# Twelve inverse sets of one pair of chunks each, all split over partitions, in place of two split sets and five whole ones

## What is computed

```python
for t in range(S):
    y[:, :, t] = np.einsum('bhd,bhde->bhe', rt, state)
    Sa = np.einsum('bhde,bhe->bhd', state, at)
    state_decay = state * wt[:, :, None, :] - np.einsum('bhd,bhe->bhde', Sa, bt)
    state = state_decay + np.einsum('bhd,bhe->bhde', vt, kt)
```

## Time and profile before

| what | value |
|---|---|
| median of 3 runs | 884.25 us (879.71 to 886.81) |
| profiled execution | 889.22 us, its span 887.5 us |
| busy share | PE 90%, DVE 57%, ACT 44%, POOL 33% |
| POOL in the chain that ended last | 10% of the span, all ahead of 144 us |
| attention ends, gated layers start | about 450 us |

### The profile page before, as it was taken

The page is one execution under the profiler, slowest core; times in us unless marked ns, Lnnn a source line. Parts: engine busy times, 40 slices in busy tenths (PEclk is TensorE's granted clock), DMA queues, the critical chain, the costliest instruction groups (busy, mean ns, idle before and its releaser), DMA issues.

```text
span 887.5 us, 29938 instructions
## 1 busy us (share of the span) xinstructions
PE 794.7 (90%) x13477; PEld 733.7 (83%) x13477; DVE 508.2 (57%) x706; ACT 386.3 (44%) x521; POOL 291.1 (33%) x476
## 2 busy tenths in 40 slices
PE   4776887998998989788789999999999999999997
PEld 4775876887887878677678999899988999899997
DVE  5794664675665753323238658644686347853475
ACT  1223333334334334434448256731767217671374
POOL 4088894780971961840003020122002120030200
PEclk9798998899899978969999999999999999999999
DMA  9996983875795444362333000100101001010001
GB/s 114 142 137 117 115 113 84 109 105 121 95 134 88 77 115 92 86 156 41 79 87 106 1 36 1 63 1 1 37 19 45 1 0 37 19 45 1 1 1 44
DMA packets 238203, 59.10 MB, mean 67 GB/s; under 512 B 228448, under 2 KB 233468, under 8 KB 238076
## 3 DMA queue, kind: packets, MB, share of 16 engines
q1 hardware_dynamic: 160092, 43.75, 25.8%
q10 hardware_dynamic: 77984, 13.45, 11.2%
HBM read 43.01 MB, written 14.16 MB: 64 GB/s over the span
## 4 chain that ended last, share of the span: by engine, by line
PE 69%; POOL 10%; issue 6%; DVE 6%; ACT 4%; DMA 3%; ACTq 1%; SPq 1%; DVEq 0%; POOLq 0%
PE p L1045 37%; PE p L690 12%; PE p L848 3%; PE p L788 3%; POOL prod L439 3%; POOL y_t L442 3%; PE p L1137 3%; PE p L798 2%; POOL prod L456 2%; POOL t_pair L459 2%; PE p L814 2%; PE p L833 2%; PE p L711 2%; DVE stage L1340 2%; PE p L755 2%
## 5 line engine op out<-in xcount | busy, mean ns | idle before, releaser
L456 POOL TENSOR_TENSOR prod<-t_pair 128x30 f32<-128x30 f32 (+9 forms) x150 | 91.8, 612 | 92.9 <-DMA t_pair<-m_scratch 81.3
L1354 POOL TENSOR_TENSOR big<-stage,big 128x1024 fp32r<-128x1024 f32 x12 | 28.8, 2398 | 276.8 <-DVE stage L1294 276.8
L1045 PE MATMUL p<-xs,w 128*128 128x384 f32 x560 | 110.2, 335 | 0.0
L1045 PE MATMUL p<-wsg_hi,big 128*128 128x384 f32 x384 | 98.6, 335 | 2.2 <-ACT stage L1199 1.9
L1045 PEld LDWEIGHTS p<-xs,w 128*128 128x128 f32 x560 | 98.5, 188 | 0.6 <-ACT stage L1191 0.2
L1045 PE MATMUL p<-wo,big 128*128 128x320 f32 x576 | 91.4, 312 | 7.0 <-DVE big L1258 7.0
L1045 PEld LDWEIGHTS p<-wo,big 128*128 128x128 f32 x576 | 85.3, 188 | 12.3 <-DVE big L1258 11.1
L459 POOL TENSOR_TENSOR t_pair<-t_pair,prod 128x30 f32<-128x30 f32 (+9 forms) x150 | 90.2, 601 | 11.8
L1045 PEld LDWEIGHTS p<-wsg_hi,big 128*128 128x128 f32 x384 | 69.6, 188 | 3.2 <-ACT stage L1199 2.6
L616 DVE TENSOR_TENSOR ar_sb<-p,mask 128x512 f32<-128x512 f32 x24 | 16.6, 692 | 69.3 <-PE p L788 69.3
L1340 DVE SCALAR_TENSOR_TENSOR stage<-tmp,cols,stage 128x768 f32<-128x768 f32 x48 | 48.7, 1015 | 12.9 <-ACT stage L1232 12.0
(11 more groups left out here) (154 smaller groups left out, 1696.9 us busy)
## 6 DMA issues: line engine op xcount, KB each, us to landing
raw_r<-in_r_dram SPq DMA_DIRECT2D x48, 80.0 KB, 3.7
vp<-in_v_dram ACTq DMA_DIRECT2D x96, 40.0 KB, 2.6
x_scratch<-y_t ACTq DMA_DIRECT2D x48, 80.0 KB
out_dram<-stage SPq DMA_DIRECT2D x11, 320.0 KB, 2.3
m_scratch<-n_t SPq DMA_DIRECT2D x48, 64.0 KB
t_pair<-m_scratch SPq DMA_DIRECT2D x5, 512.0 KB, 4.8
t_scratch<-t_pair SPq DMA_DIRECT2D x5, 512.0 KB, 3.9
t_sb<-t_scratch SPq DMA_DIRECT2D x20, 128.0 KB, 2.7
```

Of the source, the lines that this page charges most:

```text
L456: pool.tensor_tensor(p_v, tp[:, 0:s, s:s + 1].to_broadcast([PAIRS, s, n]), tp[:, s:s + 1, s + 1:C].to_broadcast([PAIRS, s, n]), ALU.mult). ...
L1045: last = pe.matmul(out_of(p, half), l, r, start=step == 0 and first, stop=step == steps - 1 and not part)
L1354: pool.tensor_tensor(dst, src, hi.bitcast(F32), ALU.subtract).then_inc(sem_, 1)
```

## The change

Every set is now a split one with one pair of chunks: `SETS` is 12, `set_of(u)` is (u // 2, u % 2), and set g belongs to chunks 2g and 2g+1. Sets take turns in two buffers of `t_pair`, of a new `t_half` (the rows that a partition updates), of `t_sb`, and in two halves of each DRAM scratch. SP no longer loads the halved rows from DRAM; POOL copies them out of `t_pair` with two copies of 64 partitions x 512 elements at the head of each set. The two whole-matrix loads of sets 0 and 1 stay as they are; from set 2 on, a set g+2 is loaded right behind the way of set g into `t_sb`, in step 2g+7. In the steps up to 6, SP loads w (ahead of b), and the first such load of a comes behind the load of set 0. The wait of DVE ahead of the first write of `y_t` is gone.

```diff
-        SPLIT = 2
-        SETS = NU // 4 + 1
+        SETS = NU // 2
+        ELIM = [(2 * (C - 2) + 4) * g for g in range(SETS + 1)]
...
-            def next_pair(u):
+            def next_wkb(u):
                 if u % 2 == 1 and u // 2 + 2 < NU // 2:
+                    if u < R_LAG:
+                        sp.wait_ge(w_full, u + 1)
+                        load(w, "w", u // 2 + 2, w_in)
...
+            def load_set(g):
+                sp.wait_ge(m_out, 64 * (g + 1))
+                for half in range(2):
+                    sp.dma_start(t_pair[half * HP:(half + 1) * HP, g % 2], in_scratch(m_pairs, g)).then_inc(m_in, 16)
+
+            def next_a(u):
+                if u % 2 == 1 and u // 2 + 2 < NU // 2:
                     sp.wait_ge(a_full, u + 1)
                     load(a, "a", u // 2 + 2, a_in)
...
-                    if g and at == 0:
-                        sp.wait_ge(m_in, M_IN[g])
+                    if g >= 2 and at == 0:
+                        sp.wait_ge(m_in, M_IN[g - 1])
...
+                    if at == 1 and g < 2:
+                        load_set(g)
+                    if u == 1:
+                        next_a(u)
...
                     sp.wait_ge(elim, ELIM[g + 1])
-                    if g:
-                        sp.wait_ge(t_in, g * 64)
+                    if g >= 2:
+                        sp.wait_ge(t_in, T_IN[g - 1])
+                    for half in range(2):
+                        sp.dma_start(in_scratch(t_pairs, g).rearrange("n (i x) t -> x n i t", x=2)[half],
+                                     t_half[half * HP:(half + 1) * HP, g % 2]).then_inc(t_out, 16)
...
+                    if g + 2 < SETS:
+                        load_set(g + 2)
...
-            for g in range(SPLIT):
+            for g in range(SETS):
+                mine, pivot = t_half[:, g % 2], t_pair[:, g % 2]
+                done = ELIM[g]
                 pool.wait_ge(m_in, M_IN[g + 1])
+                if g >= 2:
+                    pool.wait_ge(t_out, T_OUT[g - 1])
+                for half in range(2):
+                    rows = slice(half * HP, (half + 1) * HP)
+                    if done:
+                        pool.wait_ge(elim, done)
+                    pool.tensor_copy(mine[rows], pivot[rows, half:C:2, :]).then_inc(elim, 1)
+                    done += 1
...
-            for g in range(SPLIT, SETS):
...
-                if un is not None and un % 2 == 1 and un // 2 + 2 < NU // 2:
-                    load_side(w, "w", un // 2 + 2, w_in)
+                uw = un if c is not None else u if u == R_LAG else None
+                if uw is not None and uw % 2 == 1 and uw // 2 + 2 < NU // 2:
+                    load_side(w, "w", uw // 2 + 2, w_in)
...
-                    if cy == 0:
-                        dve.wait_ge(t_out, T_OUT[SPLIT])
-                    elif cy % 2 == 0:
+                    if cy and cy % 2 == 0:
                         dve.wait_ge(y_out, 16 * 4 * (cy // 2))
```

More of the change, by code:

```diff
@@ L45, in attention_memory @@
         t.r_t = sb("r_t", [P, RR, 2, 4, 2, 2, 2, C])
-        t.t_sb = sb("t_sb", [P, 2, 4, 2, 4, C])
+        t.t_sb = sb("t_sb", [P, 2, 2, 2, 4, C])
+        t.t_half = sb("t_half", [P, 2, C // 2, C])
         t.vp = sb("vp", [P, RV, 2, H, HP])
@@ L151, in attention_part @@
     e_inv, e_end, e_t, a_t, kb_t, kb_n, n_t, r_t = mem.e_inv, mem.e_end, mem.e_t, mem.a_t, mem.kb_t, mem.kb_n, mem.n_t, mem.r_t
-    t_pair, prod, t_sb, vp, x_sb, z, s_sb, vp_t = mem.t_pair, mem.prod, mem.t_sb, mem.vp, mem.x_sb, mem.z, mem.s_sb, mem.vp_t
+    t_pair, t_half, prod, t_sb = mem.t_pair, mem.t_half, mem.prod, mem.t_sb
+    vp, x_sb, z, s_sb, vp_t = mem.vp, mem.x_sb, mem.z, mem.s_sb, mem.vp_t
     ar_sb, y_t, ident, mask = mem.ar_sb, mem.y_t, mem.ident, mem.mask
@@ L203, in attention_part @@
         y_out = sem("y_out")
-        SPLIT = 2
-        SETS = NU // 4 + 1
[L206 to L210, removed]
+        SETS = NU // 2
+        ELIM = [(2 * (C - 2) + 4) * g for g in range(SETS + 1)]
+        T_OUT = [32 * g for g in range(SETS + 1)]
+        M_IN = [32 * g for g in range(SETS + 1)]
+        T_IN = [64 * g for g in range(SETS + 1)]
         m_pairs = m_dram.rearrange("n c s t -> (n c) s t")
@@ L228, in set_of, with in_scratch @@
         def set_of(u):
[L230 to L236, removed]
+            return u // 2, u % 2
         def first_chunk(g):
-            return 2 * g if g < SPLIT else 4 * (g - SPLIT) + 4
-        def half_rows(g, rows=slice(0, P)):
-            return free(y_t[rows], g * (C // 2) * C, [[C, C // 2], [1, C]])
+            return 2 * g
+        def in_scratch(scratch, g):
+            return scratch[g % 2 * HP:g % 2 * HP + HP]
         def last_use(u):
@@ L436, in _ @@
                     p_v = prod[:, 0:m * n].rearrange("p (j t) -> p j t", t=n)
-                    if done:
-                        pool.wait_ge(elim, done)
-                    pool.tensor_tensor(p_v, t_half[:, 0:m, s:s + 1].to_broadcast([P, m, n]),
-                                       t_pair[:, g % 2, s:s + 1, s + 1:C].to_broadcast([P, m, n]), ALU.mult).then_inc(elim, 1)
+                    pool.wait_ge(elim, done)
+                    pool.tensor_tensor(p_v, mine[:, 0:m, s:s + 1].to_broadcast([P, m, n]),
+                                       pivot[:, s:s + 1, s + 1:C].to_broadcast([P, m, n]), ALU.mult).then_inc(elim, 1)
                     pool.wait_ge(elim, done + 1)
-                    pool.tensor_tensor(t_half[:, 0:m, s + 1:C], t_half[:, 0:m, s + 1:C], p_v, ALU.add).then_inc(elim, 1)
+                    pool.tensor_tensor(mine[:, 0:m, s + 1:C], mine[:, 0:m, s + 1:C], p_v, ALU.add).then_inc(elim, 1)
                     done += 2
@@ L445, in _ @@
                     pool.wait_ge(elim, done + half)
-                    pool.memset(free(y_t[half * HP:(half + 1) * HP], g * (C // 2) * C + half, [[C + 2, C // 2]]), 1.0).then_inc(elim, 1)
-            for g in range(SPLIT, SETS):
-                tp = t_pair[:, g % 2]
-                pool.wait_ge(m_in, M_IN[g + 1])
-                done = ELIM[g]
-                for s in range(1, C - 1):
-                    n = C - 1 - s
-                    p_v = prod[:, 0:s * n].rearrange("p (j t) -> p j t", t=n)
-                    pool.wait_ge(elim, done)
-                    pool.tensor_tensor(p_v, tp[:, 0:s, s:s + 1].to_broadcast([PAIRS, s, n]),
-                                       tp[:, s:s + 1, s + 1:C].to_broadcast([PAIRS, s, n]), ALU.mult).then_inc(elim, 1)
-                    pool.wait_ge(elim, done + 1)
-                    pool.tensor_tensor(tp[:, 0:s, s + 1:C], tp[:, 0:s, s + 1:C], p_v, ALU.add).then_inc(elim, 1)
-                    done += 2
-                pool.memset(tp.rearrange("p s t -> p (s t)")[:, ::C + 1], 1.0).then_inc(elim, 1)
+                    pool.memset(mine[half * HP:(half + 1) * HP].rearrange("p i t -> p (i t)")[:, half::C + 2], 1.0).then_inc(elim, 1)
         @block.scalar
```

41 lines of the change are left out of this document (10 added, 31 removed).

## The result

The changed kernel takes 885.33 us, median of 20 runs (882.87 to 889.07), beside 881.95 us for the kernel before (20 runs, 876.05 to 886.81) on the same chip: a ratio of 1.0044 with a 95% interval of 1.0025 to 1.0063. It is slower, by 3.4 us between the medians and 3.9 by the ratio, about half of the 7.3 forecast. The profiled execution took 883.02 us, its span 881.2. The kernel before, profiled again beside the experiments, took 884.25; that execution is called the second profile of the kernel before.

A forecast was written before the change was run, and what follows sets the result against it. POOL bounds up to step 12, then PE's pace; changed, POOL's chain bounds the tail: 40.7 + 12 x 27.4 + 55.4 = 424.9, plus 8.8 gives step 30 at 433.7, 7.3 us later; 884.25 + 7.3 is 891.5, range 878 to 904.

The forecast's parts named there:

- Undisturbed set: POOL's time for one split set without disturbance by DVE: 26.2 us, with the two copies 27.4.
- Copies: Two POOL copies of 512 elements at the head of each set: 1.2 us for both with gaps, upper end 2.8.
- the second rival: Head of each set in POOL's chain: copies cost what two-input sums cost, 19 us more, 911; chance 0.15.
- Full lock: POOL beside DVE's scans: POOL loses all 4.2 us a step, 18 us more over seven sets, 910; chance 0.10.
- the third rival: POOL blocked for the whole of DVE's scans: seven sets lose 8.4 us instead of 5.8, 910; chance 0.10.
- Fourth rival: DMA engines fill up: share about 0.95; past 1, late inputs cost each pair a microsecond or two, 900; chance 0.05.
- First rival: POOL keeps ahead and PE sets the pace, step 12 at 143.1: 8.9 us less, 875.4; chance 0.20.
- the length of the twelve sets in the sum: POOL's chain from its start to the last set's end: twelve sets of 27.4 us plus 55.4 of disturbance.
- The disturbance by DVE: POOL operations slowed beside DVE's with SBUF inputs: 5.8 us a set in sets 2 to 8, 55.4 in all.
- POOL's start: Start of POOL's first set: 40.7 instead of 45.0, by 2.9 us from moved w loads and 1.4 from fewer DMAs.
- The way out: From issuing the last set's transfer out of POOL to step 30's T product: 8.8 us, as before.
- The rest of the program shifts as a whole, so 884.25 + 7.3: Everything after step 30's T product moves 7.3 us later with it, giving 891.5; the profiled execution would be 896.5.

The follow-up runs named there:

- the second execution: The changed kernel run again with no edit: 885.51 us beside 882.09 for the kernel before, ratio 1.0055, profiled 887.17.
- the kernel before with its cut: The kernel before with half of the elimination left out in sets 3 to 6: 880.57 us beside 881.92, ratio 0.9990.

## Why the prediction was right in kind and too high in size

**What held.** POOL's chain became the bound; the front gained and the tail gave it back; sets follow without a pause at 31.8 to 33.6 us in the middle; PE waits for T by several us in steps 26, 28 and 30. *Undisturbed set*: 27.2 against 27.4. *Copies*: 1.28 for both with gaps against 1.2, so the second rival is refuted, and doubling the copies shows what it would have cost. *Full lock*: sets 2 to 8 lose 4.6 to 6.4 us each over 27.2, 2.3 to 3.2 a step, where the third rival has 4.2; refuted. The Trainium skill (SBUF — State Buffer, Who interferes with whom) has the later of the two operations fully blocked; read for a POOL that is always first to wait it would give the 4.2, and no set of this trace shows more than 3.2. *Fourth rival*: the DMA share was 0.79 in 80 to 145 us, where the kernel with all halves loaded has 0.90, and inputs held PE only twice between 40 and 440 us, for 3.5 and 0.9 us. (In 45 to 66 us the share was 1.06, but before it was 1.05 there too.) *First rival*: PE's own pace did not set the end; it was right about step 12, at 144.53 against its 143.1.

**The step that failed: the length of the twelve sets in the sum, 12 x 27.4 + 55.4 = 384.2 us.** It measured 376.7 and 376.9 in the two executions, 7.4 us less. The disturbance by DVE was put too high, and by less the undisturbed set. In the first execution the last set was to end at 424.9 and ended at 415.7. Of these 9.2 us

- 1.8 lie in POOL's start, 38.94 in place of 40.7, which is within what executions differ by: the second has 41.08. The term was right in its total and not in its parts: of 2.9 us forecast for the write of unit 1 only 1.7 came, since SP was busy with loads until 30.98, not 29.9; from that write to the issue of the load another 0.6 were gained; and the load of the set saved 3.7 in place of 1.4 (in the second execution 1.6). Putting w back on ACT left the start where it was;
- 2.8 lie in the undisturbed sets: the 376.7 us of all twelve less their losses are 27.16 each, 0.24 less than the 27.4 forecast;
- 4.6 lie in the disturbance, 50.8 against 55.4: set 0 1.4 less, set 1 1.4 more, sets 2 to 8 1.8 less, sets 9 to 11 2.8 less. (Summed as the prediction did it, each operation's time above the shortest of its shape.) The last three sets lost 3.7, 1.8 and 1.3.

The way out took 7.8, not 8.8, so the T product of step 30 came at 423.47 in place of 433.7, **10.2 us earlier**; in the second execution, with start and way out as forecast, at 426.85, 6.9 earlier.

**A second step that failed, with the opposite sign: "The rest of the program shifts as a whole, so 884.25 + 7.3".** The 7.3 were measured against one execution whose PE pace was slow (step 30 at 426.36; 422.23 in the second profile). A bound by POOL doesn't depend on PE's pace, so its time was to be reckoned absolutely: 433.7 and the 462.9 that follow step 30 in that execution make 896.6 for the forecast's own chain. By that sum the error is 13.6 against the profiled 883.02, of it 10.2 ahead of step 30 and 3.3 behind it, where the executions of this study took between 459.5 and 462.9. The prediction had this number, 896.5, and set it aside as that execution's luck. Adding the difference to the median instead hid about half of the error: against a kernel before of ordinary pace, the same chain stands 11.5 us behind in step 30 (433.7 against 422.23), not 7.3. So the forecast came as near as it did partly by luck.

**The reading behind it.** I took the earlier trace rows, 32.7 us a pair, as PE's own pace and so put POOL's bound in the tail alone. With POOL cut in sets 2 to 11 PE goes at 30.9 (31.1 in the kernel before with its cut), less than the 32.4 to 33.6 that POOL's sets 2 to 7 take, and doubled copies lengthen steps 12 to 24 by some 9 us. Leaving out work in the tail alone brings 3 us, in sets 2 to 11 14. So POOL's chain costs time from about step 12 on. That all 14 us are T coming late is not shown: the kernels with loaded halves kept a pace of 31.6 to 33.3 us a pair with T mostly early. It changes the picture, not the sum, as that was made from POOL's chain.

**Smaller points.** The load of a held PE 3.49 us, not 1 or 2, beside POOL's first set; with w on ACT it did not come and the time was the same, so harmless, as said. SP was never late with a set after the first.

## What to carry to other kernels

When a change makes one engine's chain the bound, reckon its end in absolute time from that chain, and only then compare with the median; a difference against a single execution of a kernel bound by another engine takes in that execution's luck. An even pace without waits doesn't show that an engine sets it: lengthen and shorten the other engine's work and see whether the pace follows. When transfers are traded for copies or back, place each by stretch: here copies pay in the first two sets, at the crowded front, and transfers behind them.

## What the runs showed of the chip beyond that

Operations of DVE with both inputs in SBUF are stretched by POOL too, and less by its shorter ones. Eleven scans of 145 to 327 us, in the second profile of the kernel before and in the changed kernel (busy, mean ns):

```profile
L648 DVE TENSOR_TENSOR_SCAN r_scan<-w_back,stage 128x512 f32<-128x512 f32 x11 | 15.0, 1361 | 0.0
L621 DVE TENSOR_TENSOR_SCAN e_scan<-w_fore,stage 128x512 f32<-128x512 f32 x11 | 14.1, 1281 | 0.0
```

```profile
L609 DVE TENSOR_TENSOR_SCAN e_scan<-w_fore,stage 128x512 f32<-128x512 f32 x11 | 13.9, 1261 | 0.0
L634 DVE TENSOR_TENSOR_SCAN r_scan<-w_back,stage 128x512 f32<-128x512 f32 x11 | 13.6, 1233 | 0.0
```

With half of POOL's work gone from the kernel before `e_scan` takes 1214 ns and `r_scan` 1240. POOL's copy of 512 elements on 64 partitions took 0.60 us at the least, 1.17 ns an element; the Trainium skill (GPSIMD Engine Reference, Engine selection) calls one-input operations roughly line rate, and the trace agrees in that two-input sums cost twice as much (2.4 ns); no run here shows the line rate itself. The changed kernel, bound by POOL, has its 20 runs within 6.2 us of each other, the kernel before within 10.8. That fits a chain on POOL that is steadier than PE, whose T product, the same 64 matmuls, takes 0.79 us or 1.29 from one step to the next as its granted clock moves: 1.00 of full speed (2.4 GHz) in steps 10 and 27 of the changed kernel, 0.50 (1.2 GHz) in steps 26 and 30, which stand behind waits for T of 3.73 and 3.62 us. Step 24 of the kernel before has 0.50 with no wait right ahead of it, and what moved it there was not settled.
